# The turned blocks go to their features' partitions by way of a scratch tensor in DRAM

## What is computed

```python
# a causal convolution whose 7 weights come per token and head (8 heads of 24 features)
w = softmax(weight_gen, axis=-1)                   # [2, 4096, 8, 7]
y[b, s, h, g] = sum_k w[b, s, h, k] * x_pad[b, s + k, h, g]
# a first MLP, 192 -> 2048 -> 192
h = np.maximum(y @ w_in, 0.0);  y1 = (h * h) @ w_out
# a second MLP of the same size
h = y1 @ w_in2;  out = (h * np.clip(h + 3.0, 0.0, 6.0) / 6.0) @ w_out2
```

## Time and profile before

| | |
|---|---|
| median of 3 runs | 1186.26 us (1185.88 to 1187.44) |
| the profiled execution's time | 1185.75 us |
| its span, first to last instruction | 1183.8 us |
| TensorE, matmuls | 1156.9 us busy, 98% |
| VectorE | 922.4 us, 78% |
| ScalarE | 672.9 us, 57% |
| granted TensorE clock, mean | 0.998 |
| DMA, mean over the span | 31 GB/s |

### The profile page before, as it was taken

The page is one execution under the profiler, slowest core; times in us unless marked ns, Lnnn a source line. Parts: engine busy times, 40 slices in busy tenths (PEclk is TensorE's granted clock), DMA queues, the critical chain, the costliest instruction groups (busy, mean ns, idle before and its releaser), DMA issues.

```text
span 1183.8 us, 26942 instructions
## 1 busy us (share of the span) xinstructions
PE 1156.9 (98%) x10412; PEld 979.0 (83%) x10412; DVE 922.4 (78%) x1054; ACT 672.9 (57%) x772; POOL 3.7 (0%) x11
## 2 busy tenths in 40 slices
PE   7999999999999999999999999999999999999998
PEld 7999998887878878787887878878788787879997
DVE  8888796886968779697886968869687796976565
ACT  6886655556555565555556455565554655556554
POOL 1000000000000000000000000000000000000000
PEclk9999999999999999999999999999999999999999
DMA  7211002002020010201002020020200202000001
GB/s 211 78 62 53 5 1 58 7 11 53 0 59 5 19 45 3 57 4 52 12 7 57 0 56 8 10 54 0 58 6 13 50 2 58 0 18 10 1 14 28
DMA packets 79440, 36.84 MB, mean 31 GB/s; under 512 B 59697, under 2 KB 76207, under 8 KB 79405
## 3 DMA queue, kind: packets, MB, share of 16 engines
q1 hardware_dynamic: 79404, 36.35, 12.1%
HBM read 24.89 MB, written 6.29 MB: 26 GB/s over the span
## 4 chain that ended last, share of the span: by engine, by line
PE 66%; SPq 15%; DVE 7%; issue 5%; ACT 4%; DMA 3%; DVEq 0%; ACTq 0%
PE h_ps L910 31%; PE y_ps L921 21%; PE y_ps L930 14%; SPq L326 10%; SPq L331 4%; DVE hid L702 3%; ACT hid L444 3%; DMA stage<-stage 2%; DVE acc L610 1%; DVE prod L632 1%; DVE hid_lo L711 1%; ACT xt L478 1%; DVE stage L645 1%; DMA stage<-in_moe_w_out_dram 0%; DMA outs<-in_x_dram 0%
## 5 line engine op out<-in xcount | busy, mean ns | idle before, releaser
L910 PE MATMUL h_ps<-xt,win 64*128 64x512 f32 (+1 forms) x4860 | 1049.6, 379 | 0.6 <-DVE wout L677 0.6
L910 PEld LDWEIGHTS h_ps<-xt,win 64*128 64x128 f32 x4860 | 814.1, 185 | 80.4 <-DVE wout L677 1.0
L921 PE MATMUL y_ps<-hid_hi,wout 64*128 64x512 f32 (+1 forms) x2160 | 566.6, 380 | 15.5 <-DVE hid L702 15.2
L460 ACT ACTIVATE hid_hi<-hid 128x1024 fp32r<-128x1024 f32 (+1 forms) x244 | 256.3, 1051 | 322.0 <-DVE hid L702 157.3
L921 PEld LDWEIGHTS y_ps<-hid_hi,wout 64*128 64x128 f32 x2160 | 383.8, 185 | 57.4 <-DVE hid L702 19.2
L711 DVE TENSOR_TENSOR hid_lo<-hid,hid_hi 128x1024 fp32r<-128x1024 f32 (+1 forms) x270 | 313.2, 1160 | 143.5 <-ACT hid_hi L460 137.4
L930 PE MATMUL y_ps<-hid_lo,wout 64*128 64x512 f32 (+1 forms) x1080 | 325.5, 381 | 0.0
L921 PE MATMUL y_ps<-hid_lo,wout 64*128 64x512 f32 (+1 forms) x1080 | 322.7, 378 | 0.0
L930 PE MATMUL y_ps<-hid_hi,wout 64*128 64x512 f32 (+1 forms) x1080 | 322.4, 378 | 0.0
L921 PEld LDWEIGHTS y_ps<-hid_lo,wout 64*128 64x128 f32 x1080 | 195.1, 185 | 18.0 <-DVE hid_lo L711 0.2
L930 PEld LDWEIGHTS y_ps<-hid_hi,wout 64*128 64x128 f32 x1080 | 195.2, 185 | 17.7
(11 more groups left out here) (87 smaller groups left out, 333.8 us busy)
## 6 DMA issues: line engine op xcount, KB each, us to landing
xwin<-in_x_dram SPq DMA_DIRECT2D x14, 960.0 KB
stage<-stage SPq DMA_DIRECT2D x312, 16.0 KB, 1.8
out_dram<-outs SPq DMA_DIRECT2D x240, 16.0 KB, 1.6
out_dram<-outs SPq DMA_DIRECT2D x240, 8.0 KB, 1.4
stage<-in_moe_w_out_dram SPq DMA_DIRECT2D x8, 384.0 KB, 5.9
stage<-in_moe_w_in_dram SPq DMA_DIRECT2D x4, 512.0 KB, 5.1
stage<-in_moe_w_in_dram SPq DMA_DIRECT2D x8, 256.0 KB, 5.3
wraw<-in_weight_gen_dram SPq DMA_DIRECT2D x16, 112.0 KB, 2.0
```

What stands on the lines that cost most here:

```text
L460: act.activation(hi, hid[:, slot, :, 0:width], ACT.Copy).then_inc(hi_done, 1)
L910: return pe.matmul(h_ps[:, s % 2, t, 0:tokens.stop - tokens.start], win[layer][r, wn, cols], src[r, xn, tokens], start=bool(rows) and n in ...
L921: return pe.matmul(ps[:, 0, tokens], wout[layer][r, tile, w_cols], src, start=bool(rows) and s == 0 and n == 0, stop=not rows and s == STE ...
```

## The change

`move_blocks` no longer goes from SBUF to SBUF. It waits for the second transpose (`turn_rest`), writes `blocks` with four DMAs, one for each block row, into a new tensor `by_feature` in DRAM of 192 features x 512 tokens, where each piece of 128 tokens (512 bytes) goes to its feature's row, waits until all four have landed (`blocks_out`), and reads the tensor back with two DMAs, 128 rows of 2 KB into `xs_main` and 64 rows of 2 KB into `xs_rest`. The wait for `x1_lo` (the low parts of the chunk before are made, so `xs_main` and `xs_rest` are free) stands ahead of the reads now, and the wait for the first transpose is gone. ScalarE's two waits count one DMA per chunk in place of 16 and 8.

```diff
--- before.py
+++ after.py
@@ -100,6 +100,8 @@
     out_rows = out.rearrange("(p r) d -> p (r d)", r=ROWS)
     out_blocks = out.rearrange("(b t r) (f q) -> f t b r q", b=PBLOCKS, t=Q, q=Q)
     x_flat = x.rearrange("b s d -> (b s d)")
+
+    by_feature = nc.dram_tensor("by_feature", [D, N], fp32, kind="Internal").ap()
 
     ctx = ExitStack()
     with ctx:
@@ -190,6 +192,7 @@
         x2_lo = sem("x2_lo")
         o_copied = sem("o_copied")
         o_added = sem("o_added")
+        blocks_out = sem("blocks_out")
         x_main_moved = sem("x_main_moved")
         x_rest_moved = sem("x_rest_moved")
         out_turned = sem("out_turned")
@@ -319,17 +322,14 @@
 
             def move_blocks(c):
 
+                sp.wait_ge(prep_done, prep_value(c, "turn_rest"))
+                for b in range(PBLOCKS):
+                    sp.dma_start(by_feature.rearrange("(f t) (b n) -> b t f n", t=Q, b=PBLOCKS)[b],
+                                 blocks[b * Q:(b + 1) * Q, :].rearrange("t (f n) -> t f n", n=P)).then_inc(blocks_out, 16)
+                sp.wait_ge(blocks_out, 16 * PBLOCKS * (c - (VECTOR - 1)))
                 sp.wait_ge(x1_lo, 2 * c + 4)
-                sp.wait_ge(prep_done, prep_value(c, "turn_main"))
-                for f in range(P // Q):
-                    for b in range(PBLOCKS):
-                        sp.dma_start(xs_main[f * Q:(f + 1) * Q, b * P:(b + 1) * P],
-                                     blocks[b * Q:(b + 1) * Q, f * P:(f + 1) * P]).then_inc(x_main_moved, 16)
-                sp.wait_ge(prep_done, prep_value(c, "turn_rest"))
-                for f in range(REST // Q):
-                    for b in range(PBLOCKS):
-                        sp.dma_start(xs_rest[f * Q:(f + 1) * Q, b * P:(b + 1) * P],
-                                     blocks[b * Q:(b + 1) * Q, N + f * P:N + (f + 1) * P]).then_inc(x_rest_moved, 16)
+                sp.dma_start(xs_main, by_feature[0:P, :]).then_inc(x_main_moved, 16)
+                sp.dma_start(xs_rest, by_feature[P:D, :]).then_inc(x_rest_moved, 16)
 
             def store_turned(c):
 
@@ -472,9 +472,9 @@
             def split_moved_hi(c, dst, free):
 
                 act.wait_ge(mm1_done, free)
-                act.wait_ge(x_main_moved, 16 * PBLOCKS * (P // Q) * (c - (VECTOR - 1)))
+                act.wait_ge(x_main_moved, 16 * (c - (VECTOR - 1)))
                 act.activation(dst[:, 0, :], xs_main, ACT.Copy).then_inc(x1_hi, 1)
-                act.wait_ge(x_rest_moved, 16 * PBLOCKS * (REST // Q) * (c - (VECTOR - 1)))
+                act.wait_ge(x_rest_moved, 16 * (c - (VECTOR - 1)))
                 act.activation(dst[REST:P, 3, :], xs_rest, ACT.Copy).then_inc(x1_hi, 1)
                 act.wait_ge(x1_hi, 2 * c + 6)
                 act.activation(dst[0:REST, 2, :], dst[REST:P, 3, :].bitcast(fp32), ACT.Copy).then_inc(x1_dup, 1)
```

## The result

The kernel after takes 1168.15 us (median of 4 runs, 1165.54 to 1170.75), against 1186.85 us before. The ratio is 0.984, with a 95% interval of 0.982 to 0.987: 18.7 us faster. The profiled execution took 1165.54 us, the shortest of the four, with a span of 1163.8 us; it is 20.2 us under the one of before.

The account below looks back on a forecast made before the run. TensorE, busy 1156.9 of 1183.8 us, bounds the kernel; 24 DMAs issued on one queue stall it in thirteen chunks. Profiled 1185.75 us minus 18.3 gives 1167.4, on the median's scale 1168.0 us; 8-in-10 range 1166 to 1172 us.

Parts of the forecast that it names:

- The chain and its price: One queue's issue of 24 DMAs makes step 14's relu 3.5 us late; 1.36 us lost per chunk, 18.3 us overall.
- The three waits: ScalarE at line 478 35.3 us, VectorE at line 692 26.5 us, TensorE for line 702's gate 15.2 us; thirteen times each.
- The forecast of 18.3 us: Recovery from the stalls of thirteen chunks at step 14: 12 x 1.36 + 1.93 = 18.3 us.
- The terms of the round trip: After the second transpose: writes' issue 2.0 us, landing 2.3, reads' issue 0.8, landing 2.8; rest there at 549.2 us.
- The free time at step 14: ScalarE's copies back to back bring the relu 2.62 us sooner; TensorE needs 1.36 us of that, 1.26 us to spare.
- limit of 14.6 us: Time between the transposes' end and the rest's last harmless landing at 555.94 us; the transfers need about 8 us.
- Rival B: Stall goes, but TensorE keeps the tail's pace of 4.434 us a step: 3.7 us come back, 1171.7 us; chance 0.06.
- A's own range: Full recovery of the stalls, the forecast itself: 1168.0 us, own range 1166.5 to 1169.5 us; chance 0.78.
- Rivals C: Round trip takes 14.6 to 16.0 us, late but less than the moves: 1177 us in the middle; chance 0.05.
- D: Writes cost by the piece, 3.8 us issue each; rest lands 4.5 us later than now: 1245 us; chance 0.06.
- E: Something else holds step 14, or earlier window load and stores disturb the data: nothing gained, about 1186 us; chance 0.05.

Follow-up runs that it names:

- GpSimd's moves: Kernel before, its 24 moves kept, with the 8 moves of the rest issued by GpSimd's queue instead of SP's: 1169.72 us, ratio 0.986.
- late split: Kernel before, its 24 moves kept, with the splits of moved tokens put behind the relu and the gate of step 14: 1170.11 us, ratio 0.986.
- slowed kernels: Kernel after with each of the four writes made five times (20 writes), 1175.05 us, or seven times (28 writes), 1256.19 us.
- ten executions of after: Kernel after, unchanged, run again for its spread; with the first four, ten times: 1165.36, 1165.54, 1166.85, and seven from 1169.24 to 1170.75 us.
- both remedies: Kernel after with the splits also put behind the relu and the gate of step 14: 1169.44 us, ratio 0.986.
- 128-byte pieces: Kernel after with each write cut into 768 pieces of 128 bytes in place of 192 of 512: 1169.44 us, ratio 0.986.
- a wait per iteration: Kernel after with TensorE waiting for its own last matmul at the start of each of 14 main-loop iterations: 1171.26 us, ratio 0.987.

## Why the prediction was right

**The chain and its price** held. The three waits of the earlier trace rows were one chain. GpSimd's moves leave the bytes on their old route, and none of the three is left. The late split leaves ScalarE's wait (7.9 us of 35.3) and takes away what stood behind it. The forecast of 18.3 us is what was won from the stalls, within what the pace hides: from the profiled execution of before to that of after it is 20.2 us, of which about 1.5 us are pace (before ran four of its chunks and its tail at 4.43 us a step, some 80 steps x 0.018; the profiled execution of after none).

**The terms of the round trip** were a little high, to no effect: writes 0.45 us each (0.49), landing 2.0 us (2.3), the reads' landing 3.0 and 3.1 us (2.8), together 6.9 us where I had 7.9. The Trainium skill (DMA: Bandwidth & Descriptors, "Anatomy of one DMA — SWDGE (gpsimd) path") puts most of a fixed 2.0 us per DMA down to the wait for the write's receipt; the estimate from its fit, which is for the other issue path, was 2.9 us for each trip. The trace has 2.0 us out, below that, and 3.1 us back, near it; how much of either is the receipt no run shows. Both fall into the 14.6 us that are free.

**The free time at step 14** came out to 0.01 us in its first term: the relu 5.33 us after its predecessor, forecast 5.32, and chunk 2 had shown that TensorE doesn't notice. The limit of 14.6 us was 0.65 us too generous for data that come together: the prediction took it from the rest alone, though the main part's copy stands first. Only the slowed kernels could feel that.

**Rival B was underrated.** I gave 0.06 to a pace of 4.434 us. It is the usual one, by the times of seven of ten executions of after. I took the pace for something that varies from chunk to chunk; in before it does, and it changes back to 4.416 only behind a restart. Without stalls the slower pace, once there, stayed to the end in every profile. Its price was off as well: I put the 3.7 us on top of 1168.0, but 1168.0 already held before's own slow chunks. The two real cases are about 1165.4 and 1169.2 to 1170.8 us. The median of the first four, 1168.15, happens to fall between them, next to the forecast of 1168.0. That it came so near is luck: over all ten it is 1169.4 us, at the upper end of A's own range (five of the ten times lie outside that), and inside the 1166 to 1172 that were given for 8 in 10.

**Rivals C, D and E** fell: the landing is 7 us inside the limit, the issue of a write takes 0.45 us, and nothing else holds step 14.

## What to carry to other kernels

When an engine works in a written order, ask of each wait who is queued behind it: here a relu lost 3.5 us to data that only the next iteration needed, and moving the copies and subtractions behind the relu and the gate was worth as much, within the spread, as rebuilding the transfer. Many small DMAs on one queue cost their issue, 0.63 us each here, and can be made fewer by a detour through DRAM if the two landings in series (some 5 us) fit into the time that is free; work that time out first, part by part in the order in which the data are taken. And a longer stall can have a steeper price, when TensorE's granted clock falls: 1.1 us of idle time at a clock of 1.00 cost 1.4, 4.3 us with a clock of 0.50 behind it cost 6.8 on average (88 / 13).

## What the runs showed of the hardware

TensorE has two paces for the same instructions at the same granted clock, 4.416 and 4.434 us for a step of 38 matmuls of half height. In seven profiles with no stalls at step 14, but for the 0.3 us of the late split (after three times, the late split, GpSimd's moves, both remedies, the 128-byte pieces), the main loop has one of them from about 145 us on, six times the slower. A change from 4.434 back to 4.416 was only seen behind a stall or a forced restart (in before, with 20 and 28 writes, with a wait per iteration). The change to 4.434 also came with no wait near it (in before at about 1112 us, behind the last stall, and in the places named above). It isn't the same as the two halves of the rows loading their weights in step: the late split does so behind chunk 3 and keeps the slower pace, before does so and mostly has the faster. What makes the pace change is open; a change late in a run would account for the one time of 1166.85 us, of which there is no profile.

TensorE's course can repeat itself to 0.001 us over a thousand us: two executions of after and one of the kernel with both remedies do, apart from a constant shift.

The issue of a move from SBUF to SBUF took 0.63 us for 32 pieces of 512 bytes, that of a write to DRAM 0.45 us for 192 of them and 0.67 us for 768 of 128 bytes: the number of pieces is the small part of it. GpSimd issued the same moves in 0.51 us each.
